# A flag loaded in each round against a count held in a register: the loops over expert tiles of a routed expert layer

## What is computed

```python
x = attention(q, k, v)          # linear attention: exp-normalised q and k, 8 heads of 64
u = x + (relu(x^T w_tok1) w_tok2)^T
x = u + relu(u w_ch1) w_ch2     # the mixer
for b, s in tokens:             # the routed experts, 8 of them
    e = argmax(x w_gate) if s == 0 or sigmoid(x w_local) < 0.5 else previous e
    out[b, s] = softmax(x w_gate)[e] * (relu(x w1[e]) w2[e])
```

## Time and profile before

| | |
|---|---|
| time, median of 3 runs | 794.91 us (794.33 to 796.45) |
| the profiled execution's own time | 790.27 us |
| its span, first to last instruction | 788.6 us |
| TensorE matmuls busy | 749.5 us, 95% |
| VectorE, ScalarE, GpSimd busy | 316.6, 234.1, 142.4 us |
| mean granted TensorE clock | 0.991 of full speed |

### The profile page before, as it was taken

The page is one execution under the profiler, slowest core; times in us unless marked ns, Lnnn a source line. Parts: engine busy times, 40 slices in busy tenths (PEclk is TensorE's granted clock), DMA queues, the critical chain, the costliest instruction groups (busy, mean ns, idle before and its releaser), DMA issues.

```text
span 788.6 us, 14829 instructions
## 1 busy us (share of the span) xinstructions
PE 749.5 (95%) x4836; PEld 678.5 (86%) x4837; DVE 316.6 (40%) x611; ACT 234.1 (30%) x409; POOL 142.4 (18%) x162
## 2 busy tenths in 40 slices
PE   6999999999999999999999999996999999997993
PEld 6879999999999999999999999874888888875882
DVE  6746241225332235332225424762522622257450
ACT  3743042023132023133021141313422522255340
POOL 6562020002020002020000023111221221211220
PEclk9999999999999999999999999999999999999998
DMA  9932122012131012100010510105360620136400
GB/s 210 378 66 59 33 68 54 1 32 61 31 81 41 1 32 62 31 21 11 1 35 1 196 62 16 62 28 190 118 230 34 211 90 26 36 134 210 155 27 2
DMA packets 69514, 61.80 MB, mean 78 GB/s; under 512 B 51484, under 2 KB 53244, under 8 KB 69472
## 3 DMA queue, kind: packets, MB, share of 16 engines
q1 hardware_dynamic: 65952, 51.77, 22.2%
q0 software_dynamic: 3520, 9.44, 3.5%
HBM read 52.99 MB, written 10.31 MB: 80 GB/s over the span
## 4 chain that ended last, share of the span: by engine, by line
PE 80%; DVE 6%; issue 3%; DMA 3%; POOL 2%; ACT 2%; SPq 2%; DVEq 1%; ACTq 0%; POOLq 0%
PE bank L572 36%; PE bank L718 13%; PE bank L693 12%; PE bank L514 5%; PE bank L543 4%; POOL qb L1577 2%; PE bank L705 2%; PE bank L537 2%; PE bank L486 2%; DMA x_rows<-x1n 1%; PE bank L593 1%; PE bank L502 1%; PE bank L582 1%; PE bank L524 1%; PE bank L641 1%
## 5 line engine op out<-in xcount | busy, mean ns | idle before, releaser
L572 PE MATMUL bank<-u_h,wc_h 128*128 128x288 f32 x384 | 120.0, 312 | 1.5 <-DVE hid_l L1303 1.5
L718 PE MATMUL bank<-wslots,hT_h 128*128 (+1 forms) x336 | 107.5, 401 | 10.1 <-DVE hT_l L1470 10.1
L572 PE MATMUL bank<-hid_h,wc_h 128*128 128x288 f32 x384 | 117.0, 305 | 0.0
L693 PE MATMUL bank<-wslots,xgT_h 128*128 (+1 forms) x344 | 111.8, 406 | 4.2 <-DVE wslots L1454 3.1
L572 PE MATMUL bank<-hid_l,wc_h 128*128 128x288 f32 x384 | 113.2, 295 | 0.0
L572 PE MATMUL bank<-u_l,wc_h 128*128 128x288 f32 x384 | 113.1, 295 | 0.0
L572 PE MATMUL bank<-u_h,wc_l 128*128 128x288 f32 x384 | 113.0, 294 | 0.0
L572 PE MATMUL bank<-hid_h,wc_l 128*128 128x288 f32 x384 | 113.0, 294 | 0.0
L1303 DVE SCALAR_TENSOR_TENSOR hid_l<-bank,hid_h 128x288 fp32r<-128x288 f32 x96 | 43.3, 454 | 132.4 <-ACT hid_h L872 132.2
L718 PEld LDWEIGHTS bank<-wslots,hT_h 128*128 128x128 f32 x336 | 62.1, 191 | 23.5 <-issue 10.8
L693 PEld LDWEIGHTS bank<-wslots,xgT_h 128*128 128x128 f32 x344 | 61.0, 188 | 17.9 <-issue 7.0
(11 more groups left out here) (236 smaller groups left out, 1090.2 us busy)
## 6 DMA issues: line engine op xcount, KB each, us to landing
w1raw<-in_moe_w_dram SPq DMA_DIRECT2D x24, 512.0 KB, 4.6
w2raw<-in_moe_w_dram SPq DMA_DIRECT2D x24, 512.0 KB, 6.4
wc_raw<-in_moe_w_ch_dram SPq DMA_DIRECT2D x8, 768.0 KB, 11.2
x_rows<-x1n SPq DMA_DIRECT2D x24, 192.0 KB, 2.1
kb<-in_k_dram SPq DMA_DIRECT2D x24, 144.0 KB, 3.1
qb<-in_q_dram SPq DMA_DIRECT2D x24, 144.0 KB, 3.1
vb_e<-in_v_dram SPq DMA_DIRECT2D x16, 144.0 KB, 3.6
vb_o<-in_v_dram SPq DMA_DIRECT2D x16, 144.0 KB, 3.4
```

What stands on the lines that cost most here:

```text
L572: last = pe.matmul(to, lhsT, rhs, start=(m == 0), stop=(m == len(mms) - 1))
L693: last = pe.matmul(bank[half][:, :], xgT[a][:, c, :], w1s[x][:, bass.ds(n & 1, 1), c, half * 512:(half + 1) * 512].rearrange("p a n -> p ( ...
L718: last = pe.matmul(bank[5][:, :], hT[a][:, f, :], w2s[x][:, bass.ds(n & 1, 1), f, :].rearrange("p a n -> p (a n)"), start=(f == 0 and (a, ...
```

## The change

Each of the four loops loads the number of tiles in use once, ahead of the loop, and compares the loop's index with it. POOL's load of the same number moves from behind its loop to ahead of it. SyncE's loop and the tables are as they were.

```diff
+            n = pe.value_load(tiles[0:1, 0:1], min_val=1, max_val=NT)
             with pe.Fori(EARLY, NT) as t:
-                live = pe.value_load(table[0:1, 3, bass.ds(t + 1, 1)], min_val=0, max_val=1)
-                with pe.If(live):
+                with pe.If(t < n):
                     tile(t, again=True)
...
+            n = act.value_load(tiles[0:1, 0:1], min_val=1, max_val=NT)
             with act.Fori(EARLY, NT) as t:
-                live = act.value_load(table[0:1, 3, bass.ds(t + 1, 1)], min_val=0, max_val=1)
-                with act.If(live):
+                with act.If(t < n):
                     tile(t, again=True)
...
+            n = dve.value_load(tiles[0:1, 0:1], min_val=1, max_val=NT)
             with dve.Fori(EARLY, NT) as t:
-                live = dve.value_load(table[0:1, 3, bass.ds(t + 1, 1)], min_val=0, max_val=1)
-                with dve.If(live):
+                with dve.If(t < n):
                     tile(t, again=True)
...
+            n = pool.value_load(tiles[0:1, 0:1], min_val=1, max_val=NT)
             with pool.Fori(EARLY, NT) as t:
-                live = pool.value_load(table[0:1, 3, bass.ds(t + 1, 1)], min_val=0, max_val=1)
-                with pool.If(live):
+                with pool.If(t < n):
                     tile(t, True)
 
-            n = pool.value_load(tiles[0:1, 0:1], min_val=1, max_val=NT)
             pool.wait_ge(x_in, 16 * n + 32)
             pool.wait_ge(rows_stored, 16 * n)
```

## The result

| | before | changed |
|---|---|---|
| median | 794.93 us (794.03 to 796.45, 6 runs) | 789.72 us (786.07 to 792.27, 6 runs) |
| ratio | | 0.9928, 95% interval 0.99 to 0.9956 |
| span of the profiled execution | 788.6 us | 784.5 us |
| mean granted TensorE clock | 0.991 | 0.993 |

The changed kernel is faster by 0.7%, 5.2 us between the medians; 4.4 us were forecast. The two profiled executions differ by 4.1 us.

The account below looks back on a forecast made before the run. TensorE's matmuls bound the kernel until they end, then POOL's sequencer holds the end; 3.84 us for empty rounds plus 0.55 for the count's load made 4.4 us, so 794.91 became 790.5 us, range 788.9 to 795.2.

Parts of the forecast that it names:

- What bounds the kernel, and where it doesn't: Whole kernel: TensorE busy 749.5 of 788.6 us; other engines count only where it waits or has ended.
- The value 0 for the loads that the chain listed in the exposed rounds: ScalarE's L1021 and VectorE's L1531, 698 to 735 us: run while their engine works, so no gain.
- Empty rounds, 6 x 0.64 = 3.84 us: POOL's six rounds past the last tile: each loses its flag load and followers, 0.64 us, 3.84 us in all.
- The load of the number of tiles, 0.55 us: Behind POOL's loop: moving this load to the loop's entry, where POOL has idle time, gains 0.55 us.
- The landing next: Kernel's end: the last scatter's landing at 780.0 binds next, so no more than 4.5 us can be had.
- VectorE at 779.1, TensorE at 777.6: Kernel's end: both engines finish their empty rounds then, ahead of POOL's drain at 780.3.
- The drain has a fixed end: Rival at POOL's DRAIN: started 4.4 us sooner it grows as much, 794.9 us, 17%; partly, 792.9 us, 8%.
- The change does not shorten a round: Rival in the loops: compare costs what the load did, or loads issue another way; 794.9 us, 2%.
- more than the end: Rival in the two exposed rounds: loads are in the path, up to 2.0 us more gain, 788.5 us, 8%.
- back edges fetch their code: Rival in TensorE's loop: shifted code makes each back edge fetch again, 10 us slower, 800.5 us, 4%.
- The remark on a load's price: Seven loads: the skill's floor of about 600 ns gives an estimated 4.2 us; the rows decide.
- The sum against the median: Whole kernel: the same 4.4 us taken from the median 794.91 us gives 790.5 us, or 0.55%.

Follow-up runs that it names:

- all_but_pool: Kernel before with the change in the TensorE, ScalarE and VectorE loops, POOL's loop left as before; median 794.15 us, ratio 0.9991.
- pool_only: Kernel before with the change in POOL's loop alone, the other engines loading a flag each round; median 790.54 us, ratio 0.9941.
- pool_double: Kernel before with the flag loaded twice in each of POOL's rounds; median 798.26 us, ratio 1.005.
- load_moved: Kernel before with only POOL's load of the number of tiles moved ahead of its loop; one run, 794.7 us.
- ends_at_n: Changed kernel with the four loops ending at the held count, so no empty rounds; median 790.41 us, ratio 0.9948.
- ends_and_wait: Changed kernel with loops ending at the held count and the wait for the last scatter moved from POOL to VectorE; median 788.86 us, ratio 0.9935.
- the second: Changed kernel once more, beside the kernel before on the same chip; median 791.02 us beside 794.81 us, ratio 0.9948.
- wait_on_dve: Changed kernel with the wait for the last scatter's landing moved from POOL to VectorE; median 789.93 us, ratio 0.994.
- sp_count: Changed kernel with a held count in place of the flag load in SyncE's loop too; median 784.60 us, ratio 0.9872.
- sp_lean: Changed kernel with SyncE's loop using a held count and loading the expert's number only where the expert changes; median 781.97 us, ratio 0.9838.
- all_three: Changed kernel with loops ending at the count, the scatter wait on VectorE, and SyncE's lean loop; median 778.75 us, ratio 0.9797.

## Why the prediction was right

*What bounds the kernel, and where it doesn't.* That an operation counts only where TensorE waits or has ended held throughout. The rounds in use gave nothing: `all_but_pool` gained nothing clear of the spread, `pool_only` as much as the whole change, and the same matmuls from 698 us to the end are 77.2 us apart in both kernels. The value 0 for the loads that the chain listed in the exposed rounds was right. That they ran while their engine was at work is the reason that fits; no run moved one of them into a pause.

*Empty rounds, 6 x 0.64 = 3.84 us.* A little too high: they gave 6 x (1.03 - 0.44) = 3.5 us. The removed group was sized rightly: from the start of its first instruction to the start of the `If` are 0.64 us in the trace of before, 0.55 us for the load and its two followers (`pool_double`) and 0.09 for the address. The step that was off is that the `If` costs what it did. The compare of two registers has a MOVE in front that the listing of the built program doesn't show, 29 ns and its gap, 0.06 us a round; six of them are the 0.3 us that were missing.

*The load of the number of tiles, 0.55 us.* It gave 0.56 (`load_moved`). The sum of both terms was 4.4 us forecast and is 4.1 us.

*The landing next.* The drain was forecast at 780.3 and came at 780.7 (780.6 without the later start), the wait for the scatter at 780.1 and came at 780.4. It was met with 0.3 us to spare and not 0.1. `ends_at_n` shows the point at which it binds. VectorE is late in `pool_only` as the prediction feared (787.7 there, POOL's drain from 784.9), and the drain does outlast it.

*VectorE at 779.1, TensorE at 777.6.* They came at 779.5 and 777.7; both have the MOVE as well.

*The drain has a fixed end* (17%, and 8% for a part). Refuted: 3.664 to 3.667 us in eight of the kernels with starts from 2.6 to 10.2 us behind the scatter. The suspicion that such a long instruction waits for something was sound in part: in `ends_and_wait` it seems to wait for POOL's last instruction, and in the kernel before that was over long before. What fills the 3.66 us is open; no run here changed it.

*The change does not shorten a round*, *more than the end*, *back edges fetch their code*: the rounds are shorter, TensorE's rounds are 12.37 us as before (the chain's L718 at 566.30 and 578.67), and the profile's page counts 30 fetches in both kernels.

*The remark on a load's price.* By the floor of about 600 ns for a tensor_load that the Trainium skill gives (DMA: Bandwidth & Descriptors, section Latency and other measured facts), the seven groups are an estimated 4.2 us. The rows make them 6 x 0.64 + 0.56 = 4.4 us, and 4.1 once the MOVEs are taken off. The TENSOR_LOAD itself is 0.29 us on POOL, under that floor; only with the instructions that come with it does it come to 0.55 to 0.64 us.

*The sum against the median.* The 4.4 us were taken from the median as they stood. Between the medians were 5.2 us in the first comparison and 3.8 in the second, with the executions of the last section as the likely reason. That the figure for the median came out so near has some luck in it.

## What to carry to other kernels

A load into a register cost POOL's sequencer about 0.55 us here, 0.64 with its address, and such a load costs kernel time only where an engine's sequencer is what the end, or a stalled engine, waits for: look for it behind the last output and ahead of the first transfer of a phase, by source line, since neither busy times nor groups of instructions show it. A loop that runs to a worst-case count has its empty rounds behind its last full one; where it is the last thing in the kernel, nothing covers them. And if POOL drains last, let another engine wait for the last landing: the two need not run one behind the other. That pays only where POOL really waits for the landing: 1.5 us without empty rounds (6.5 to 4.9 us behind the scatter), under 0.1 us with them (`wait_on_dve`).

## What the runs showed of the hardware

*POOL's drain.* At the end of each of these kernels POOL's DRAIN takes 3.66 to 3.68 us, counted from the end of its last instruction or from its own start, whichever is later. ScalarE's, TensorE's and VectorE's took 7 to 17 ns where the engine had nothing left to do, SyncE's about 0.12 us. In `ends_at_n`, where TensorE's sequencer reaches its drain while matmuls are still queued, the same instruction takes 2.7 us on TensorE, to 779.6 us, where the last matmul ends too; on VectorE it takes 0.6 us with the last `yo` in work:

```profile
L80 PEldq DRAIN  x1: 2698/2698/2698, 776.9 to 776.9; - x1
L80 ACTq DRAIN  x1: 314/314/314, 777.2 to 777.2; - x1
L80 DVEq DRAIN  x1: 601/601/601, 780.0 to 780.0; - x1
```

*Two executions of one program, 5.2 us apart.* The two profiled executions of the changed kernel have spans of 784.5 and 789.8 us and the same distances at the end. Busy time by stretch, first the one with 784.5 (the number behind the last engine's busy time is the granted clock as a share of the full 2.4 GHz):

```profile
16.00:24.00 8.00, 6.33 (x55) 5.70 (x54) 6.59 (x8) 3.60 (x7) 4.62 (x3) 1.00 1.08 267
458.00:465.00 7.00, 6.45 (x48) 6.45 (x49) 2.19 (x5) 1.54 (x5) 0.00 (x0) 1.00 0.10 28
...
724.00:728.00 4.00, 4.00 (x23) 3.22 (x21) 4.00 (x4) 2.92 (x5) 0.00 (x0) 1.00 0.94 305
```

and the one with 789.8:

```profile
16.00:24.00 8.00, 6.33 (x46) 5.82 (x44) 5.65 (x6) 3.61 (x7) 4.63 (x3) 0.79 1.08 270
458.00:465.00 7.00, 4.42 (x23) 4.19 (x22) 1.28 (x3) 1.60 (x4) 0.00 (x0) 0.78 0.17 55
...
724.00:728.00 4.00, 3.79 (x9) 2.65 (x10) 1.21 (x2) 0.97 (x2) 0.00 (x0) 0.59 0.00 0
```

In three places the second one had TensorE at the lower level, 1.2 GHz, for 3.4 us (from 18.2, 461.9 and 724.7 us), and the first did not. What that cost is read from the same matmuls in both traces: 1.6 us at the first place, 1.5 at the second, and 0.7 at the third, where a shorter wait for weights behind it gave a part back. That is 3.9 of the 5.2 us. Another 1.0 us is no matter of the clock. Ahead of the second place TensorE waited longer, as the groups of instructions from 455 to 465 us and from 456 to 467 us say:

```profile
L572 PE MATMUL bank<-u_h,wc_h 128*128 128x288 f32 x21 | 6.3, 300 | 1.5 <-DVE hid_l L1303 1.5
```

```profile
L572 PE MATMUL bank<-u_h,wc_h 128*128 128x288 f32 x18 | 6.1, 337 | 2.6 <-DVE hid_l L1303 2.6
```

In the same views ScalarE (L855) waits 3.3 and 4.3 us for a transfer of `x_rows`, which is 1.0 us again. Both have a further stretch of 6.8 us at the lower level behind the 6 to 7 us for which TensorE stands still for weights; where that gap is short or gone (`sp_count`, `sp_lean`, `all_three`) there is none. This is how a first comparison of two kernels can be 1 us off: of its six runs of the changed kernel, two came at 786.1 and 786.3 us, with a mean clock of 0.993, and four at 789.2 to 792.3, with 0.987. Which executions get these stretches was not settled; a distance between two events that lie behind TensorE's last matmul, as from the scatter to the end, is free of them.
